# When the second expert's weights are loaded and split, and two pieces inside a single tile

## The reference

```python
def _moe2_ref(x, w_gate, w_output_gate, w1, w2):
    logits = x @ w_gate
    e_idx = np.argmax(logits, axis=1)
    gate_w = probs[np.arange(N), e_idx]          # softmax of the logits
    eom = 1.0 / (1.0 + np.exp(-(x @ w_output_gate)))
    for e in range(E):
        mask = e_idx == e
        h = np.maximum(x[mask] @ w1[e], 0.0)
        ye = h @ w2[e]
        out[mask] = gate_w[mask, None] * eom[mask, e, None] * ye
```

## Time and profile before

| what | us |
|---|---|
| median of 3 runs | 1141.16 |
| lowest and highest | 1140.4, 1143.56 |
| the profiled execution | 1135.01 |
| its span | 1133.3 |
| PE busy in it | 1106.1 |
| DVE, ACT, POOL busy | 623.1, 401.3, 207.4 |
| granted TensorE clock, mean | 0.997 of full speed |

### The profile page before, as it was taken

How to read it: one execution, slowest core, us unless ns; L and a number is a source line. 1 busy time by engine, 2 the same in 40 slices (tenths; PEclk the granted TensorE clock), 3 DMA queues, 4 the chain that set the end, 5 groups by cost and what they waited for, 6 DMA issues and landing times.

```text
span 1133.3 us, 18114 instructions
## 1 busy us (share of the span) xinstructions
PE 1106.1 (98%) x6514; PEld 895.9 (79%) x6515; DVE 623.1 (55%) x1364; ACT 401.3 (35%) x751; POOL 207.4 (18%) x298
## 2 busy tenths in 40 slices
PE   5999999999999999999999999999999999989997
PEld 2777777777777777777777889989998989878895
DVE  6584484674754854845744566673343336366342
ACT  3444334334434433443344355241121124244121
POOL 1000011020020020110110303532232232333222
PEclk9999999999999999999999999999999999999999
DMA  9398197394692890930130301691111122545111
GB/s 337 115 297 245 57 295 213 123 310 132 186 310 71 247 301 27 307 101 1 38 75 8 124 1 39 149 266 55 56 49 44 37 75 70 168 96 145 40 37 40
DMA packets 73007, 149.85 MB, mean 132 GB/s; under 512 B 11231, under 2 KB 12511, under 8 KB 72928
## 3 DMA queue, kind: packets, MB, share of 16 engines
q1 hardware_dynamic: 59696, 115.34, 35.3%
q0 software_dynamic: 13248, 33.71, 9.8%
HBM read 131.11 MB, written 92.01 MB: 197 GB/s over the span
## 4 chain that ended last, share of the span: by engine, by line
PE 87%; DVE 6%; DMA 3%; ACT 2%; issue 2%; POOLq 0%; POOL 0%; SPq 0%; DVEq 0%; ACTq 0%
PE bank L501 27%; PE bank L503 26%; PE bank L502 26%; PE bank L534 3%; PE bank L552 1%; DMA raw<-w_dram 1%; PE bank L568 1%; DMA s_in<-rows_dram 1%; DVE w_lo L1313 1%; PE bank L576 1%; PE bank L512 1%; ACT w_hi L967 1%; PE bank L541 1%; DVE g_buf L1176 1%; DMA XT<-xT_in_dram 1%
## 5 line engine op out<-in xcount | busy, mean ns | idle before, releaser
L501 PE MATMUL bank<-wout_lo,gT_hi 128*128 128x512 f32 x544 | 215.9, 397 | 0.0
L503 PE MATMUL bank<-wout_hi,gT_hi 128*128 128x512 f32 x544 | 212.3, 390 | 0.0
L502 PE MATMUL bank<-wout_hi,gT_lo 128*128 128x512 f32 x544 | 212.0, 390 | 0.0
L1176 DVE TENSOR_TENSOR g_buf<-g_buf,bank 128x512 f32<-128x512 f32 (+1 forms) x144 | 94.2, 654 | 107.5 <-ACT g_buf L927 107.4
L501 PE MATMUL bank<-xgT_lo,w_hi 128*128 128x256 f32 x512 | 144.8, 283 | 2.9 <-DVE w_lo L1313 2.6
L503 PE MATMUL bank<-xgT_hi,w_hi 128*128 128x256 f32 x512 | 143.8, 281 | 0.0
L502 PE MATMUL bank<-xgT_hi,w_lo 128*128 128x256 f32 x512 | 143.8, 281 | 0.0
L1180 DVE TENSOR_TENSOR gT_lo<-g_buf,gT_hi 128x512 fp32r<-128x512 f32 (+1 forms) x144 | 95.4, 662 | 72.9 <-ACT gT_hi L933 71.4
L927 ACT ACTIVATE g_buf<-bank 128x512 f32<-128x512 f32 (+1 forms) x144 | 82.5, 573 | 147.1 <-PE bank L503 145.6
L933 ACT CAST gT_hi<-g_buf 128x512 fp32r<-128x512 f32 (+1 forms) x144 | 85.9, 597 | 136.5 <-DVE g_buf L1176 136.5
L403 POOL DMA_INDIRECT rows_dram<-y_buf,row_i x34 | 35.0, 1031 | 542.0 <-DVE row_i L1270 534.4
(11 more groups left out here) (216 smaller groups left out, 1697.3 us busy)
## 6 DMA issues: line engine op xcount, KB each, us to landing
rows_dram<-x_in_dram SPq DMA_DIRECT2D x17, 4128.0 KB, 25.2
xq<-rows_dram POOLq DMA_DIRECT2D x88, 128.0 KB, 2.8
raw<-w_dram SPq DMA_DIRECT2D x20, 512.0 KB, 7.8
raw<-w_dram SPq DMA_DIRECT2D x10, 1024.0 KB, 11.1
X<-x_in_dram SPq DMA_DIRECT2D x8, 1024.0 KB, 12.4
XT<-xT_in_dram SPq DMA_DIRECT2D x7, 1024.0 KB, 5.6
win<-w_in_dram SPq DMA_DIRECT2D x4, 1024.0 KB, 11.9
y_buf<-w_out_dram POOLq DMA_DIRECT2D x6, 512.0 KB, 6.2
```

What stands on the lines that cost most here:

```text
L501: pe.matmul(o, l_hi, r_lo, start=first, stop=False)
L502: pe.matmul(o, l_lo, r_hi, start=False, stop=False)
L503: return pe.matmul(o, l_hi, r_hi, start=False, stop=last)
L1176: dve.tensor_tensor(g_buf[:, n, 0:w], g_buf[:, n, 0:w], up_b[n][:, 0:w], ALU.max).then_inc(g_ready, 1)
```

## The change

It has four parts. (1) In the first expert's program the next weights are split where `i == split_at`, and for the first expert `split_at` is a new table entry, the smaller of 2 and its last step; for the others it is their first step, as before. Here that is step 2 in place of step 1. (2) SP waits for `rows_in` 240, so also for the rows of step 2, before it loads those weights. (3) In a single tile that is the splitting step, ACT copies piece 0 behind its first `hT_hi` and piece 1 behind its second `h_rows`, and DVE subtracts both between its two `hT_lo`; pieces 2 to 7 stay where they were. (4) POOL's loop over v is written out 8 times; the first step of an expert is the end of the one before, kept in a register, and the first expert's column comes from a register too.

```diff
@@ build
+        CTL_SPLIT = 45
@@ block.sync
-            sp.wait_ge(rows_in, 160)
+            sp.wait_ge(rows_in, 240)
@@ block.gpsimd
-            with pool.Fori(0, E) as v:
-                first, end = load_ctl(pool, v + CTL_POOL, MAXP, 1), load_ctl(pool, v + CTL_POOL + 1, MAXP, 1)
-                col0 = load_ctl(pool, v + 17, COLS)
+            first, col0 = 1, pool.snap(first_col + 4)
+            for v in range(E):
+                end = load_ctl(pool, v + CTL_POOL + 1, MAXP, 1)
+                if v > 0:
+                    col0 = load_ctl(pool, v + 17, COLS)
                 with pool.If(first < end):
                     with pool.Fori(first, end) as sent:
...
+                        send_step(sent, first, col0)
+                first = end
@@ block.scalar
-            def hidden_rows(i):
+            def hidden_rows(i, piece):
                 for j in range(2):
                     act.wait_ge(h_ready, F2 * i + 4 * j + 1)
                     act.activation(h_rows[:, 4 * P * j:4 * P * j + 4 * P], h_b[j][:, :], ACT.Relu).then_inc(h_hi_done, 1)
+                    if j == 1:
+                        piece(1)
                     act.wait_ge(h_ready, F2 * i + 4 * j + 4)
                     act.copy(hT_hi[:, 4 * j:4 * j + 4, 0:P], h_b[2 + j][:, :].rearrange("p (f t) -> p f t", f=4)).then_inc(h_hi_done, 3)
+                    if j == 0:
+                        piece(0)
...
-                    with act.If(i < first + 1):
+                        with act.If(i == split_at):
                         with act.If(c1 < c2):
-                            split_expert(v + 1, 1 - s)
+                                split_expert(v + 1, 1 - s, which)
...
                 if tiles == 2:
                     hidden_T(i)
+                    rows_hi(i + 1)
+                    pieces(range(8))
                 else:
-                    hidden_rows(i)
-                rows_hi(i + 1)
+                    hidden_rows(i, lambda n: pieces((n,)))
+                    rows_hi(i + 1)
+                    pieces(range(2, 8))
...
-            c0, c1 = load_ctl(act, 0, MAXP), load_ctl(act, 1, MAXP)
+            c0, c1, split_at = 1, load_ctl(act, 1, MAXP), load_ctl(act, CTL_SPLIT, 2, 1)
...
-                c0, c1 = c1, c2
+                c0, c1, split_at = c1, c2, c1
@@ block.vector
+                dve.tensor_scalar(ctl[:, CTL_SPLIT:CTL_SPLIT + 1], end[:, 0:1], -1.0, 2.0, ALU.add, ALU.min)
...
                 else:
                     turn_quarters(i + 1)
                     h_lo_turned(i, 0)
+                    pieces(range(2))
                     h_lo_turned(i, 1)
                 rows_lo(i + 1)
...
+                pieces(range(2 if tiles == 1 else 0, 6))
...
+                pieces(range(6, 8))
```

More of the change, by code:

```diff
@@ L463, in _, with send_step @@
             pool.wait_ge(toks_shifted, 2)
-            with pool.Fori(0, E) as v:
-                first, end = load_ctl(pool, v + CTL_POOL, MAXP, 1), load_ctl(pool, v + CTL_POOL + 1, MAXP, 1)
-                col0 = load_ctl(pool, v + 17, COLS)
+            def send_step(sent, first, col0):
+                n = pool.snap(sent + 2)
+                col = nc.s_assert_within(pool.snap(col0 + (sent - first) * 2), 0, COLS - 2,
+                                         skip_runtime_bounds_check_because="an expert has room for all tokens")
+                pool.wait_ge(pairs_clear[1], 16 * clear_in(1, PAIRS))
+                pool.wait_ge(s_taken, n)
+                load_rows(col)
+                next_tokens(n)
+                pool.wait_ge(slots_in, 16)
+                pool.wait_ge(toks_shifted, n)
+                pool.tensor_copy(tok_next[:, :], slot_tok[:, bass.ds(col, 2)]).then_inc(toks_kept, 1)
+                scatter(n)
+            first, col0 = 1, pool.snap(first_col + 4)
[3 more added lines that the diff above has]
+                    col0 = load_ctl(pool, v + 17, COLS)
                 with pool.If(first < end):
                     with pool.Fori(first, end) as sent:
[L470 to L480, removed]
+                        send_step(sent, first, col0)
+                first = end
             total, after, after2 = load_ctl(pool, 8, MAXP), load_ctl(pool, 25, MAXP + 1), load_ctl(pool, 26, MAXP + 2)
@@ L1544, in _, with expert_step, pieces @@
             dve.tensor_copy(s_now[:, :], s_next[:, :]).then_inc(s_moved, 1)
-            def expert_step(i, tiles, first, c1, c2, v, s):
+            def expert_step(i, tiles, split_at, c1, c2, v, s):
+                def pieces(which):
+                    if v + 1 < E:
+                        with dve.If(i == split_at):
+                            with dve.If(c1 < c2):
+                                split_expert(v + 1, 1 - s, which)
                 if tiles == 2:
@@ L1571, in expert_step @@
                 dve.tensor_copy(s_now[:, :], s_next[:, :]).then_inc(s_moved, 1)
-                if v + 1 < E:
-                    with dve.If(i < first + 1):
-                        with dve.If(c1 < c2):
-                            split_expert(v + 1, 1 - s, range(6, 8))
-            c0, c1 = load_ctl(dve, 0, MAXP), load_ctl(dve, 1, MAXP)
+                pieces(range(6, 8))
+            c0, c1, split_at = 1, load_ctl(dve, 1, MAXP), load_ctl(dve, CTL_SPLIT, 2, 1)
             for v in range(E):
@@ L1582, in _ @@
                     with dve.Fori(c0, cf) as i:
[L1583 removed]
+                        expert_step(i, 2, split_at, c1, c2, v, v % 2)
                 with dve.If(cf < c1):
[L1585 to L1586 removed]
+                    expert_step(cf, 1, split_at, c1, c2, v, v % 2)
+                c0, c1, split_at = c1, c2, c1
 def kernel(x, state, moe_w_in, moe_w_out, moe2_w_gate, moe2_w_output_gate, moe2_w1, moe2_w2):
```

14 lines of the change are left out of this document (6 added, 8 removed).

## The result

The changed kernel took 1135.79 us in the median of 9 runs (1135.08 to 1137.59), the kernel before 1140.44 beside it (1139.18 to 1143.56): ratio 0.9955, 95% interval 0.9946 to 0.9965. That is 4.65 us, more than the 3.15 forecast and more than the 0.3% bound. Measured once more, later, it was 1133.48 against 1138.59, ratio 0.9951 (0.9938 to 0.9965).

The account below looks back on a forecast made before the run. PE was busy 1106.1 of 1133.3 us, so only its standstills could be won. Gap A's 1.65 plus gap B's 1.5 made 3.15 us, taking the median from 1141.16 to 1138.0, range 1135.6 to 1140.8.

Parts of the forecast that it names:

- All that this change can win stands in these 4.75 us: PE's three gaps from 720 us to the end, 0.42% of the run, taken as the most the change could win.
- Gap A: PE's wait in step 1, 737.97 to 739.85, behind late third rows; forecast to go whole, -1.65 us.
- the walk of VectorE: Step 1: rows there by 727.5 or 728.8, turn at 731.5 taking 1.35 us, rest 5 at 732.9, before PE's 738.20.
- rival 1: More than the sum: gap B closes by 2.3 us, C goes, gap A may be larger; 1136.7, chance 0.22.
- Gap B: PE's wait between step 14 (single tile) and step 15, 2.78 us beyond the pitch; walk gave -1.6, forecast took -1.5.
- Gap C: PE's wait of 0.32 us at 1039.48 in step 16; forecast to stay unchanged.
- No wait in step 2: ScalarE's eight copies in step 2 wait for no load; VectorE's first rest of step 3, 1.4 us late, stays hidden.
- the cover of 5 us: Step 2: weights landed by 754, ScalarE comes to them at 758.9, 5 us behind the whole load.
- The branches: Six branches around pieces 0 and 1 in single tiles, 0.24 us, forecast to hide in idle time and cost PE nothing.
- That difference I take over as it is: The 6 us between the profiled execution (1135.01) and the median of the runs (1141.16), carried unchanged into the forecast.
- Rivals 2 and 4: 2: pieces in step 14 win nothing, 1139.5, chance 0.14; 4: rows late in any order, gap A stays, 1139.7, 0.05.
- Rival 3: Code's place: POOL's eight bodies and longer ScalarE and VectorE bodies wait for code, slower, 1144, chance 0.05.

Follow-up runs that it names:

- part 1 alone: Kernel before with only SP's loads waiting for rows_in 240 and the split in step 2: ratio 0.9967, once more on another chip 0.9974.
- the version with earlier pieces: Changed kernel with ScalarE copying four w1 pieces before the first h_rows and VectorE subtracting three earlier: 0.9935 of the kernel before, again 0.9944.
- the two timed parts: Kernel before with only the later loads and split in step 2 (0.9967, again 0.9974), and with only two pieces inside the single tile (0.9985).
- POOL's loop alone: Kernel before with only POOL's loop over v written out: ratio 1.0004.
- each half alone: Kernel before with loads behind the rows but the split in step 1: 1.0072; with the split in step 2 but loads as before: 1.0004.
- set on purpose: Changed kernel with idle DVE subtractions in steps 1 to 9, three runs: PE stalls of 1.52 to 1.57, 2.24 to 2.29 and 2.79 to 2.81 us.
- the split moved: Kernel before with the split in step 2 but SP's loads as before (rows_in 160): 1141.32 against 1141.47, ratio 1.0004.

## Why the prediction was right or wrong

**The forecast, 1138.0 and "within 0.3%", was wrong; the mechanism was right and a term was mis-sized.** Against its own profile the sum seems to hold, 406.62 - 403.17 = 3.45 us where 3.15 was forecast, but that is in part luck: 0.60 us of a longer step 0 hide in it. Without step 0 it is 4.05 us: 2.01 from steps 1 and 2 (1.65 forecast) and 1.89 from step 14 (1.5 forecast). And it was given as the gain of the runs, and the five profiles of before take 406.62, 407.20, 408.63, 407.22 and 409.60 us from the plan to the end, 407.85 in the mean; the two of the changed kernel 403.17 and 402.77, 402.97. The difference is 4.88 us, and the two timed ones are 4.65 and 5.11. "All that this change can win stands in these 4.75 us" was no bound either.

**Gap A, 1.65: the step that failed.** That it goes whole was right, and so was the walk of VectorE. VectorE came to the turn at 735.90, which less the 4.51 us by which step 0 ended later (729.04 against 724.53) is 731.4 (731.5 forecast). But 1.65 was the reading of one profile. In the mean of the five profiles of before, steps 1 and 2 take 47.15 us, and 44.52 in the mean of the four in the table with the loads behind the rows and a later split: 2.63. Timed, part 1 alone gave 3.35 and 3.19. What I left out is that PE's stall can be longer, and that it can bring the lower clock, together some 2 us more; and a stall costs some 0.15 us more than PE's starts show at it. I had seen the spread of the transfer (2.1 to 11.5 us) and, for the size of gap A, used it only in rival 1.

**Gap B, 1.5: mis-sized in the same way.** 1.84 us came from the pieces, where the walk gave 1.6 and I took 1.5: the handovers cost less than I walked (0.23 inside the step, not 0.3, and 0.67 left behind it, not about 1). And the 2.78 us stall was one that brings the lower clock in some executions: steps 15 and 16 take 43.98 us in the mean over before and 43.43 in both profiles of the changed kernel, 0.55 more.

2.63 + 1.84 + 0.55 = 5.0 us, against 4.88 from end to end; step 0 has 0.17 us of the difference (4.69 us in the mean of the two, 4.51 before).

**Gap C stays** was right in the changed kernel (0.35 by the starts, 0.41 in its second profile; 0.48 and 0.40 in the two profiles of before where the clock had not fallen). **No wait in step 2** was right: ScalarE with no wait for `raw`, VectorE's first rests late and unnoticed. The weights' loads began at 736.03, which less the 3.91 us of the plan is 732.1, a little behind the 730 to 731 forecast; the cover of 5 us took it. **The branches** cost nothing that could be seen; POOL's part is worth nothing in time (1.0004), as forecast.

**"That difference I take over as it is"** was the other failing. The 6 us between profile and median were no constant. The larger part, as far as the later profiles tell, stands ahead of the change and goes with the chip: the plan was closed at 720.5 to 721.1 us in four profiles on one chip (median of before there 1137.44 us), at 722.4 to 723.2 in four on a second (1139.18) and at 725.3 to 727.0 in four on a third (1141.47). Such a part is the same for both kernels, and the profile predicted from had it small (720.11). But 1.2 us of the 6 (407.85 - 406.62) was gap A and the clock, which the change removes. The spreads fit: the runs of before differ by 2.6 to 5.3 us on one chip, those of the changed kernel by 1.3 and 2.5.

**The rivals.** Rival 1 (1136.7; its own sum, 1141.16 - 4.3, gives 1136.9) came nearest in time, and for one of its reasons: gap A was larger in the runs. Its other one, that B closes by both pieces and C goes, did not happen, and did in the version with earlier pieces. Rivals 2 and 4 fell with the two timed parts. Rival 3 fell with POOL's loop alone (1.0004): at the change of expert behind step 13 POOL comes from one body to the next in 0.31 us there and in 0.32 in the changed kernel.

## What to carry to other kernels

A stall of PE is not worth its length but what follows it: here stalls of 2.16 us and more brought, in some executions, up to 1.6 us more at the lower clock, and those of up to 1.83 us did not. When a change removes a wait for a transfer on crowded queues, take the wait from several profiles and not from one, and look whether the runs spread: a spread of some us in a kernel whose work is fixed can itself be something to win. And when loads are put behind others, move their use as well: each half alone gave nothing here or cost 0.7%.

## What the runs showed of the hardware

- The granted clock fell to its lower level (0.50) behind stalls of PE of 2.16 to 2.81 us: behind all three gaps A of 2.16 to 2.33 us, behind five of ten gaps B of 2.8, and behind 3 of 9 and 6 of 9 of those set on purpose. It fell behind none of 1.52 to 1.83 us (14 of them: nine set on purpose, three of before, the ones of POOL's loop alone and of the split moved), with full use of PE on both sides. It came back to 1.00 within about 5 us of PE's going on. Of two stalls alike in one program the one had it and the other not.
- A transfer of 2 KB (`s_in`) took 11.4 to 12.2 us behind 4 MB of weights on the queues in five profiles of before, where its median is 2.4 to 2.6, and still 10.2 us at most in the changed kernel, in a place where nobody waits for it.
